# Moving the start addresses of the split second-layer weights and of the combine matrix within 512 bytes

## The reference

```python
x = attention(q, k, v)            # 4 x 8 heads x 576 x 64, window of 128, linear bias
# soft MoE with 8 experts of 4 slots
d = softmax_over_tokens(x @ phi);  slot_in = d.T @ x
slot_out[e] = relu(slot_in[e] @ w1[e]) @ w2[e]
y = softmax_over_slots(x @ phi) @ slot_out          # c @ slot_out
# second MoE: 8 experts, every token through every expert
P = sinkhorn(exp(y @ w_gate - max))                 # 8 rounds
for e in range(8):
    out += P[:, e:e+1] * (relu(y @ w1[e]) @ w2[e])  # w1 512x1024, w2 1024x512
```

## Time and profile before

| | us |
|---|---|
| median of 3 runs (lowest, highest) | 1112.82 (1112.59, 1113.67) |
| the profiled execution's own time | 1115.35 |
| span of the profile, first to last instruction | 1113.6 |
| busy in the span: PE, PEld, DVE, ACT, POOL | 1080.4, 861.3, 465.0, 327.2, 145.5 |
| granted clock of TensorE, mean | 0.971 |

### The profile page before, as it was taken

One profiled execution on the slowest core, in us unless ns is written; L12 is line 12 of the kernel. 1 busy time (PEld: TensorE's weight loads), 2 busy tenths in 40 slices (PEclk: granted clock), 3 DMA queues, 4 the chain that ended last, 5 costly groups with the idle time before them and its releaser, 6 DMA issues.

```text
span 1113.6 us, 15960 instructions
## 1 busy us (share of the span) xinstructions
PE 1080.4 (97%) x5815; PEld 861.3 (77%) x5815; DVE 465.0 (42%) x1179; ACT 327.2 (29%) x882; POOL 145.5 (13%) x218
## 2 busy tenths in 40 slices
PE   7999968799999999999999999999999999999998
PEld 5888832178888888888888888888888888888887
DVE  6766642045754243433343343334333443343331
ACT  6777612042223222321232132213221322131120
POOL 6545410012000200110021002100210021000000
PEclk9999979569999999999999999999999999999999
DMA  5773199922020202020202020202020200000111
GB/s 180 260 265 115 39 361 383 351 76 69 8 77 1 75 2 76 1 76 1 76 3 76 1 76 1 76 1 77 2 76 1 76 1 1 0 1 29 48 48 48
DMA packets 36849, 87.17 MB, mean 78 GB/s; under 512 B 2976, under 2 KB 2976, under 8 KB 36768
## 3 DMA queue, kind: packets, MB, share of 16 engines
q1 hardware_dynamic: 36768, 86.07, 21.6%
HBM read 81.35 MB, written 4.72 MB: 77 GB/s over the span
## 4 chain that ended last, share of the span: by engine, by line
PE 94%; DMA 3%; DVE 1%; ACT 1%; issue 0%; POOL 0%; SPq 0%; POOLq 0%; DVEq 0%
PE bank L681 24%; PE bank L682 24%; PE bank L683 24%; PE bank L640 6%; PE bank L482 3%; PE bank L492 3%; PE bank L511 3%; PE bank L592 2%; PE bank L624 2%; DMA slot_raw<-slot_w_in 1%; PE bank L529 1%; DMA early_raw<-slot_w_in 1%; DMA q_ring<-q_tiles 1%; PE bank L567 1%; PE bank L523 1%; PE bank L661 0%
## 5 line engine op out<-in xcount | busy, mean ns | idle before, releaser
L681 PE MATMUL bank<-w_hi,h_hi 128*128 128x512 f32 x1152 | 452.4, 393 | 0.0
L682 PE MATMUL bank<-w_lo,h_hi 128*128 128x512 f32 x1152 | 450.9, 391 | 0.0
L683 PE MATMUL bank<-w_hi,h_lo 128*128 128x512 f32 x1152 | 448.8, 390 | 0.0
L767 ACT ACTIVATE h_hi<-bank 128x384 fp32r<-128x384 f32 x384 | 157.5, 497 | 593.0 <-PE bank L640 593.0
L967 DVE SCALAR_TENSOR_TENSOR h_lo<-bank,h_hi 128x384 fp32r<-128x384 f32 x384 | 187.4, 551 | 191.9 <-ACT h_hi L767 191.6
L683 PEld LDWEIGHTS bank<-w_hi,h_lo 128*128 128x128 f32 x1152 | 216.7, 188 | 46.9
L681 PEld LDWEIGHTS bank<-w_hi,h_hi 128*128 128x128 f32 x1152 | 216.6, 188 | 45.9 <-issue 3.1
L682 PEld LDWEIGHTS bank<-w_lo,h_hi 128*128 128x128 f32 x1152 | 216.6, 188 | 40.9
L1017 DVE SCALAR_TENSOR_TENSOR acc<-bank,gate_now,acc 128x512 f32<-128x512 f32 x126 | 94.5, 750 | 299.2 <-PE bank L683 299.2
L456 POOL TENSOR_TENSOR w_lo<-w_raw,w_hi 128x512 fp32r<-128x512 f32 x56 | 71.3, 1289 | 705.4 <-ACT w_hi L746 705.4
L640 PE MATMUL bank<-c_stack,g_stack 128*128 128x384 f32 x384 | 85.4, 344 | 0.1
(11 more groups left out here) (126 smaller groups left out, 445.5 us busy)
## 6 DMA issues: line engine op xcount, KB each, us to landing
w_raw<-big_w_in SPq DMA_DIRECT2D x16, 2048.0 KB, 8.3
slot_raw<-slot_w_in SPq DMA_DIRECT2D x18, 1024.0 KB, 9.3
early_raw<-slot_w_in SPq DMA_DIRECT2D x8, 1024.0 KB, 13.7
q_ring<-q_tiles SPq DMA_DIRECT2D x18, 256.0 KB, 4.3
k_ring<-k_tiles SPq DMA_DIRECT2D x18, 256.0 KB, 4.8
v_ring<-v_rows SPq DMA_DIRECT2D x18, 256.0 KB, 2.7
out_rows<-acc SPq DMA_DIRECT2D x18, 256.0 KB, 2.0
late_raw<-slot_w_in SPq DMA_DIRECT2D x4, 1024.0 KB, 12.7
```

Source lines behind the costliest of these rows:

```text
L681: pe.matmul(to, h_hi[b][:, f, col], w2_hi[parity][:, f, :], start=(f == 0), stop=False)
L682: pe.matmul(to, h_hi[b][:, f, col], w2_lo[parity][:, f, :], start=False, stop=False)
L683: done = pe.matmul(to, h_lo[b][:, f, col], w2_hi[parity][:, f, :], start=False, stop=(f == FT - 1))
L767: act.activation(h_hi[c % 2][:, f, :], bank[H_BANK[n % H_BANKS]][:, 0:CT], ACT.Relu).then_inc(h_hi_ready, 1)
```

## The change

No instruction is added, removed or reordered. Only start addresses change. `PHASE` is 112 words, 448 bytes.

```diff
+    PHASE = 112
...
+        fold = sb("fold", [P, SLOTS])
+        fold_half = sb("fold_half", [P, 2, SLOTS])
+        sb("pad_below", [P, P - PHASE])
         c_stack = sb("c_stack", [P, TILES * P], F32R)
+        sb("pad_above", [P, P - PHASE])
         w1_raw = sb("w1_raw", [P, DT, F])
         so4 = sb("so4", [P, DT, 4, SLOTS])
         gate_sb = sb("gate_sb", [P, DT, GATES])
-        fold = sb("fold", [P, SLOTS])
-        fold_half = sb("fold_half", [P, 2, SLOTS])
...
-        w2_hi0, w2_lo0, hid_rows = place(X_AT, RAW_AT, ("w2_hi0", [P, FT, D], F32R), ("w2_lo0", [P, FT, D], F32R),
+        w2_hi0, w2_lo0, hid_rows = place(X_AT + PHASE, RAW_AT, ("w2_hi0", [P, FT, D], F32R), ("w2_lo0", [P, FT, D], F32R),
                                          ("hid_rows", [P, 512]))
-        si_rows, = place(LATE_END, RAW_AT, ("si_rows", [P, D]))
-        so_rows, = place(LATE_END, RAW_AT, ("so_rows", [P, D]))
+        si_rows, = place(LATE_END + PHASE, RAW_AT, ("si_rows", [P, D]))
+        so_rows, = place(LATE_END + PHASE, RAW_AT, ("so_rows", [P, D]))
...
-        w2_hi1, w2_lo1, h_hi1, h_lo1 = place(
-            LATE_END, END, ("w2_hi1", [P, FT, D], F32R), ("w2_lo1", [P, FT, D], F32R),
-            ("h_hi1", [P, FT, CT], F32R), ("h_lo1", [P, FT, CT], F32R))
+        w2_hi1, w2_lo1 = place(LATE_END + PHASE, END, ("w2_hi1", [P, FT, D], F32R), ("w2_lo1", [P, FT, D], F32R))
+        h_hi1, h_lo1 = place(
+            LATE_END + 2 * FT * D + P, END, ("h_hi1", [P, FT, CT], F32R), ("h_lo1", [P, FT, CT], F32R))
```

## The result

The changed kernel takes 1129.88 us (median of 4 runs, 1129.74 to 1130.25) where the kernel before takes 1112.72 in the same series: a ratio of 1.0153, 95% interval 1.0135 to 1.0170. It is slower by 17.2 us. The forecast was 1083, with 1066 to 1118 as its range, so both the sign and the range were wrong. The prediction had left its slower cases, with a chance of 0.22, out of the range.

A forecast was written before the change was run, and what follows sets the result against it. TensorE's matmul cost from start to start was taken to bound the last 876 us; -27.6 (lines 681 to 683) and -3.1 (line 640) gave -30.7 us, from 1112.8 to 1082, rounded up to 1083, range 1066 to 1118.

The forecast's parts named there:

- slower cases: Second MoE matmuls slower: by the absolute address, 1133 us, chance 0.15, or by a worse meeting, 1159 us, 0.07.
- What bounds the kernel: Last 876 us, from 237 us on: the cost of one TensorE matmul from start to start, and nothing else.
- The excess of 13.3 ns belongs to the reading of operands, not to a fixed pause: Second MoE matmuls: 226.7 ns against 213.3 for 512 columns; the excess is gone at half clock, so operand supply.
- The addresses: Modulo 512: base up 128 bytes, c_stack at 64, w2 at 192, h, g_stack and first MoE load buffers at 256.
- Part 1, lines 681 to 683: 3456 matmuls: 8 ns less each, 27.6 us gained; bounds -46 to +46 us.
- Part 2, line 640: 384 matmuls, 48 per expert: 8 ns less each, 3.1 us gained; bounds 6.7 us each way.
- Parts 3, 4 and 6: g_products and attention transposes, writers of w2 and c_stack, waits and order: 0 us; transposes at most 3.6 us either way.
- Part 5, the loads: First MoE loads, 130 to 237 us, landing 128 bytes higher: 0 us, with 3 us kept either way.
- a rival of its own at 0.03: First MoE: matmul pitch stays and loads get faster with targets at multiples of 256; 1110 us, chance 0.03.
- Nothing happens: Second MoE: the 13.3 ns belong to float32r at full clock, not to addresses; 1112.8 us within 0.2%, chance 0.29.
- The rival of the absolute address: Second MoE: extra cycles follow the moving operand's distance past 512; 233.3 ns, +20.5 us, 1133 us, chance 0.15.
- 448 is the worse meeting of the two streams: Second MoE: w2 at 448 from h makes matmuls slower, 240 ns, +46 us, 1159 us, chance 0.07.

The follow-up runs named there:

- h at 0: The kernel before with only the stationary operands h_hi and h_lo moved, by 384 bytes, to a multiple of 512; 1129.23 us, ratio 1.0144.
- all at 0: The kernel before with 384 bytes of padding ahead of ident, all large operands at a multiple of 512, relative places kept; 1110.41 us, ratio 0.9971.
- all at 192: The kernel before with 64 bytes of padding ahead of ident, all large operands 192 past a multiple of 512; 1113.75 us, ratio 1.0005.
- w2 at 384: The kernel before with only w2 (and the rows beside it) moved, by 256 bytes, so its distance to h is 256; 1113.91 us, ratio 0.9997.
- h_lo at 256: The kernel before with only h_lo moved, by 128 bytes, h_hi and w2 keeping distance 0; 1125.18 us, ratio 1.0100.

## Why the prediction was wrong, point by point

- **What bounds the kernel.** Right. TensorE's distance from start to start in the second MoE decided the result, and no other engine took over.
- **The excess of 13.3 ns belongs to the reading of operands, not to a fixed pause.** The part that the change moved does: moving the stationary operand alone changed the distance (h at 0). At half clock the distance stayed at 427 ns (426.6 before, 426.8 after). What the 13.3 ns at distance 0 are made of stays open; no distance tried brought them down.
- **The addresses.** Right, and they mattered. The distance of `w2` from `h` became 192 modulo 256, and the shift of the common base by 128 bytes, which the words of the change don't mention, is what made the loads faster.
- **Part 1, lines 681 to 683: the step that failed.** I bounded the cost at 13.3 ns either way, which holds (+6.7 measured), and then chose the sign by a picture: two streams that start together at the same place must get in each other's way. No row supported that. The runs showed the opposite: for these matmuls equal places are the best of the five distances tried. The term was put at -27.6 us and is +23.0. The settling of the earlier trace rows was the evidence that there was something to gain or lose, and it was no evidence for which. Nor did it support the size of 8 ns: the "0.22 us" that took off half of the excess is a difference of two starts that are printed to 10 ns. The trace's own records have 224 ns there, and 236 for the "240" before it. A difference of 0.22 also stands in the undisturbed stretch of the earlier trace rows, where every distance is 226 or 227 ns:

```profile
600.66 0.39 PE L682 MATMUL bank<-w_lo,h_hi 128*128 128x512 f32 x1
600.88 0.39 PE L683 MATMUL bank<-w_hi,h_lo 128*128 128x512 f32 x1
```

No distance in the earlier trace rows is below 226.7 by more than 3 ns, and their mean is above it.

- **Part 2, line 640.** The sign was right and the size near, with luck in it: -3.1 us expected, 96 x 0.03 = -2.9 us with `c_stack` moved alone. The 8 ns and their reason were those of part 1, where both failed, and only about half of the gain is in the matmuls of line 640. In the changed kernel the saving is 4.8 us, and w2 moved alone brings it too: from 361.46 to 364.96 us it has 3.50 us for the four and twelve more, the same as the changed kernel. So the two parts' gains overlap there, and 1.0162 x 0.9974 x 0.9977 = 1.0112 understates the 1.0153 of the change; without the factor of `c_stack` it is 1.0139, within the interval of 1.0135 to 1.0170.

```profile
361.46 0.87 PE L640 MATMUL bank<-c_stack,g_stack 128*128 128x384 f32 x4
...
364.96 0.39 PE L681 MATMUL bank<-w_hi,h_hi 128*128 128x512 f32 x1
```

- **Parts 3, 4 and 6.** Nothing seen of them: before 237 us the transposes' stage has 123.68 us of TensorE's time in its first 130, against 123.51 before, and VectorE and ScalarE keep their totals.
- **Part 5, the loads.** I took 0 and kept 3 us either way. With all operands moved together, 2.5 and 3.4 us less were measured (ratios 0.9977 and 0.9971), at the edge of that bound. I had given it a rival of its own at 0.03, too little for a mechanism with both a stage in which TensorE waits and a known side. The Trainium skill's sentence in "DMA: Bandwidth & Descriptors", "How a descriptor splits into AXI transactions", that a start off a multiple of 256 costs more, fits the four rows of the loads; the runs moved the write side, of which that section doesn't speak.
- **The rivals.** "Nothing happens" is refuted: h at 0 moved the weights alone and the distance went from 226.7 to 232.6 ns. The rule of the Trainium skill, "TensorE: Matmul & The Clock Gate" ("Step-by-step: what each phase is for"), that the weight load takes no read bandwidth from the running matmul, doesn't agree with this: where the weights start changes what a matmul costs. Which load costs which matmul stays open, as h_lo at 256 couldn't part them. The rival of the absolute address had the distance right to a tenth of a ns (233.3) and the cause wrong, as all at 0, all at 192 and w2 at 384 show. The remaining one, that 448 is the worse meeting of the two streams, had the cause right. I priced it at 13 ns, twice what it was, and gave it 0.07.

## What to carry to other kernels

In a dense stream of float32r matmuls of 512 columns with a weight load each, keep the moving and the stationary operand at the same place modulo 256 bytes; for the four matmuls of 384 columns in between, 64 bytes off was the faster of the two places tried, so try a few distances there. Place buffers that DMA fills in a DMA-bound stage at multiples of 256. Padding put in ahead of one tensor moves all that is stacked above it; work out every address before and after, not only the one meant. Where a trace bounds a cost on both sides of nothing and no row gives the sign, that is no basis for a forecast with a sign: the ends belong in the range, and two kernels that differ in one distance settle it.

## What the runs showed of the hardware

- A float32r matmul of 512 columns that runs beside a weight load costs 226.7 to 233.3 ns at full clock, depending on the distance between the two operands' start addresses modulo 256 bytes: 226.7 at 0, 228.9 at 64, 233.3 at 32, 128 and 192 (232.6 at 128 with h moved). At half clock both the kernel before and the changed one have 426 to 427 ns.
- Distance alone isn't all: at 128 the mean is 233.3 ns with w2 moved and 232.6 ns with h moved. Why isn't known, nor which of two meetings costs (that with the weights being loaded, or with the place of its own), nor whether a step finer than 32 bytes would do better than 0.
- The whole stream moved together by 64, 128 or 384 bytes keeps its 226.7 ns in all three cases.
- Loads of 1 MB parts into targets at a multiple of 256 bytes moved 393 to 406 GB/s between 160 and 215 us (four kernels), at 128 or 192 past a multiple of 512 they moved 380 to 389 (eleven). A 2048-byte packet took 84 and 88 ns on the median.
- After four `c_stack` matmuls of 384 columns the 512-column stream of the kernel before needs about eight matmuls to be back at 226.7 ns, with 224 to 236 ns in between; with `c_stack` moved 64 bytes it needs about five.
